# A gated linear attention: causal mask moved from TensorE to POOL, carry weights broadcast by DMA, bias halves in two PSUM banks, output gate rows loaded earlier

## The chip, the cores and the metric

The kernel runs on one core of one Trainium2 chip. The metric is the device time of one launch in microseconds (us). A core has the engines PE (TensorE, matrix products), ACT (ScalarE), DVE (VectorE) and POOL (GpSimd), the queue SP that issues most transfers, and 16 DMA engines. SBUF is its working memory with 128 partitions, PSUM holds the results of PE in eight banks.

## The reference, cut to what matters

Four batches times eight heads (32 heads in all), 768 steps, 40 columns a head. A recurrent attention with exponential gates is followed by a layer with eight experts (one per token) and a gated network. The change touches the first part alone:

```
for t in range(S):
    m_new  = maximum(f[:, :, t] + m, i[:, :, t])
    f_stab = exp(f[:, :, t] + m - m_new);  i_stab = exp(i[:, :, t] - m_new);  m = m_new
    C = f_stab * C + i_stab * outer(v[t], k[t])
    n = f_stab * n + i_stab * k[t]
    h = C @ q[t];  denom = maximum(abs(n @ q[t]), 1)
    y[t] = sigmoid(o_gate[t]) * h / denom
x = y as (3072 tokens, 320 columns)      # then experts, then the last network
```

## The kernel before

The 768 steps are cut into 6 groups of 128 (`NC`), and one chunk is one group of one batch: 24 chunks (`NT`), numbered n = 4 c + b. Inside a chunk the recurrence is written as attention: weights exp(bias) between keys and queries, times the products of q and k, times v; what came before the chunk enters through a state per head, faded by a carry weight.

**Rows.** DVE scans the gates of a group (`rows_scan`), ACT and DVE split them into high and low parts (`rows_high`, `rows_low`), SP stores them to DRAM (`rows_store`) and loads them back as operands: `bias_key` and `bias_carry` by group (`group_rows`), `bias_query` by chunk (`query_rows`). A bias product has 18 rows: the low and high key parts times ones, ones times the query parts. The rows that pick a head are a 0/1 pattern made by POOL in `bias_query[0]` and copied by ACT for the other three batches (L686).

**PE.** `front(n)`: the carry product (L1293, from the second group on) writes carry weights to the bank `CARRY`; then for each half of the heads a bias product (L1298) into the one bank `BIAS` and a product of the bf16 identity with a constant mask (L1299) that adds -1e30 where a key comes after the query; between the halves the scores (L1306). `increments(n)` (L1319) makes the new state, `head_columns(n)` (L1330) turns the outputs to tokens and makes the logits, `gate_turn(n)` (L1279) transposes the output gate rows into `BIAS`, `attend(n)` multiplies the state by qa (L1344) and v by the weights (L1353). The order by hand, turn i of the loop at L1387: front(i+1), increments(i), in one turn of four the ranks of a group, head_columns(i-1), gate_turn(i+2), attend(i). "Turn" below is this.

**ACT.** Turn i: `outputs(i-1)` copies the outputs (L679), `weights(i+1, h)` takes the exponentials of both halves (L660), `decayed` copies the last carry column (L666), `gates(i+2)` applies the gate (L672, L674).

**DVE.** Turn i: floor of the denominators of chunk i-2, `carry(i+1)` (qa = q times the carry weights in PSUM, L876), reciprocal, `scaled(i-2)` (L920, L922), `probs(i+1, 0)` (weights times scores, L883), `head_sum`, `update(i)` of the state (L896), `probs(i+1, 1)`. Every fourth turn it also scans rows, or chooses experts, or ranks.

**POOL.** Turn i: `gated_heads(i-1)` (zT, L605), `fade(i)` (L597), `weigh(i+1)` (L589), and from turn 8 on `scatter(i-8)`, which sends finished rows to DRAM in the order of the experts (L612).

**SP.** For each chunk `loads(n)` waits until chunk n-4 is done, then issues the gate rows `og_tok`, q and k, and k and v by tokens, and `query_rows(n)`; in one of four it stores and reloads the rows of a group.

The single bank `BIAS` is passed on: half 0, half 1, gate rows, each written only when ACT has read the one before (`weights_ready`, `tanh_ready`). Before the loop PE zeroes some banks, runs 14 products on constants so as to be busy (`keep_warm`), and runs front(0) and gate_turn(1).

```
def front(n):                                            # cut
    pe.wait_ge(tanh_ready, n + 1)
    for h in range(2):
        if h:
            pe.wait_ge(weights_ready, 2 * n + 1)
        mm(BIAS, bias_key, bias_query, stop=False)       # L1298
        mm(BIAS, ident16[:], maskT[:], start=False)      # L1299
        if h == 0:
            ...                                          # scores, L1306
```

## Time and profile before

| what | value |
|---|---|
| runs | 908.79, 911.25, 911.15 us; median 911.15 |
| the profiled execution | 914.29 us, its span 912.5 us, mean granted clock 0.964 |
| PE busy | 849.8 us (93%), 6301 products |
| DVE, ACT, POOL busy | 509.3, 394.0, 110.7 us |
| DMA | 109.37 MB, mean 120 GB/s |
| attention part | to about 190 us of the span |
| first bias product, last attend | 15.99 us, 184.16 us |

The span runs from the first to the last instruction of one profiled execution; 1.8 us of that execution lie around it. The executions that were only timed took up to 0.6% less. Busy times of several engines overlap. "Granted clock" is the share of 2.4 GHz that the chip let PE run at. In a timeline row the first number is the start, the second how long the instruction was busy, and brackets tell how long the engine stood idle before it and what released it.

### The profile page before, as it was taken

Reading aid. Unit: us, or ns where it says so; the run is one execution under the profiler, and the core shown is the slowest. Engines: PE = TensorE matmul, PEld = TensorE weight load, DVE = VectorE, ACT = ScalarE, POOL = GpSimd, SP = SyncE. Lnnn points to the kernel's source line nnn. Section 1 sums busy time; section 2 is a strip of 40 time slices with the busy share of each in tenths; the row PEclk is TensorE's granted clock in tenths of the full one; section 3 lists DMA queues with packets and bytes.
Section 4 is the critical chain, followed back from the end, with each engine's and each line's share of the span. In section 5 each row is a group of like instructions: output and inputs, shape, how many; then the busy total and the mean of one; then the engine's idle time right before and its main releaser. Section 6 shows DMA issues by size and latency. Waiting matters only on the chain.

```text
span 912.5 us, 18039 instructions
## 1 busy us (share of the span) xinstructions
PE 849.8 (93%) x6301; PEld 743.1 (81%) x6301; DVE 509.3 (56%) x1060; ACT 394.0 (43%) x714; POOL 110.7 (12%) x151
## 2 busy tenths in 40 slices
PE   5999999915999999999994999999999999999997
PEld 2777777615999999999993788888888888888886
DVE  4466566555788787878772344354354354453432
ACT  4444444404777767677761232232232233233122
POOL 4234454340000000000001100100100100100000
PEclk8899999966999999999997999999999999999999
DMA  6354445258889999999961100100100100100000
GB/s 166 89 146 129 147 140 165 72 200 279 251 266 262 266 269 279 264 253 291 296 203 37 30 1 1 58 1 1 58 0 0 58 0 0 58 0 2 28 1 29
DMA packets 76567, 109.37 MB, mean 120 GB/s; under 512 B 11380, under 2 KB 55284, under 8 KB 76516
## 3 DMA queue, kind: packets, MB, share of 16 engines
q1 hardware_dynamic: 72036, 98.20, 36.7%
q0 software_dynamic: 2304, 7.88, 2.6%
q10 hardware_dynamic: 2176, 2.62, 0.9%
q8 instruction: 30, 0.49, 0.2%
q14 instruction: 21, 0.17, 0.1%
HBM read 92.21 MB, written 16.47 MB: 119 GB/s over the span
## 4 chain that ended last, share of the span: by engine, by line
PE 85%; issue 5%; DMA 3%; ACT 2%; POOL 2%; DVE 1%; ACTq 1%; SPq 1%; POOLq 0%; DVEq 0%
PE psum L1419 42%; PE psum L1494 5%; PE psum L1495 5%; PE psum L1496 5%; PE psum L1443 4%; PE psum L1445 4%; PE psum L1444 4%; PE psum L1279 3%; PE psum L1330 2%; PE psum L1353 2%; PE psum L1306 2%; PE psum L1298 2%; PE psum L1299 1%; DMA w_raw<-w 1%; PE psum L1411 1%
## 5 line engine op out<-in xcount | busy, mean ns | idle before, releaser
L1242 DVE TENSOR_TENSOR gated_lo<-gated,gated_hi 128x512 fp32r<-128x512 f32 x72 | 49.9, 693 | 185.7 <-ACT gated_hi L807 185.7
L802 ACT ACTIVATE sigm_sb<-psum 128x512 f32<-128x512 f32 x72 | 43.0, 598 | 255.8 <-PE psum L1419 255.8
L1419 PE MATMUL psum<-nT_hi,w_gv_hi 128*128 128x512 f32 x432 | 125.1, 398 | 2.6 <-DVE nT_lo L1229 2.6
L1419 PE MATMUL psum<-nT_lo,w_gv_hi 128*128 128x512 f32 x432 | 124.5, 396 | 0.0
L1419 PEld LDWEIGHTS psum<-nT_lo,w_gv_hi 128*128 128x128 f32 x432 | 81.5, 189 | 19.9
L1419 PEld LDWEIGHTS psum<-nT_hi,w_gv_hi 128*128 128x128 f32 x432 | 79.0, 189 | 16.9 <-DVE nT_lo L1229 2.8
L1419 PE MATMUL psum<-nT_hi,w_gv_lo 128*128 128x512 f32 x288 | 90.6, 396 | 0.0
L635 POOL DMA_INDIRECT c_rows<-y_by_slot,slot_idx x24 | 22.8, 948 | 555.8 <-DMA y_by_slot<-y_tile 286.3
L1494 PE MATMUL psum<-w_out_hi,gated_hi 128*128 128x320 f32 x288 | 89.8, 312 | 0.0
L1495 PE MATMUL psum<-w_out_lo,gated_hi 128*128 128x320 f32 x288 | 89.1, 309 | 0.0
L1496 PE MATMUL psum<-w_out_hi,gated_lo 128*128 128x320 f32 x288 | 89.0, 309 | 0.0
L1419 PE MATMUL psum<-xT_hi,first_hi 128*128 128x256 f32 (+1 forms) x456 | 79.3, 283 | 2.0 <-DVE xT_lo L1095 2.0
L1443 PE MATMUL psum<-second_hi,hT_hi 128*128 128x320 f32 x248 | 78.4, 316 | 1.5 <-DVE hT_lo L1116 1.5
L1419 PE MATMUL psum<-xT_lo,first_hi 128*128 128x256 f32 (+1 forms) x456 | 79.1, 283 | 0.0
L1445 PE MATMUL psum<-second_hi,hT_lo 128*128 128x320 f32 x248 | 76.7, 309 | 0.0
L1444 PE MATMUL psum<-second_lo,hT_hi 128*128 128x320 f32 x248 | 76.7, 309 | 0.0
L723 ACT ACTIVATE second_hi<-w_raw 128x640 fp32r<-128x640 f32 x76 | 54.4, 737 | 36.8 <-PE psum L1445 33.6
L717 ACT ACTIVATE first_hi<-w_raw 128x1536 fp32r<-128x1536 f32 x38 | 56.6, 1490 | 29.4 <-DMA w_raw<-w 29.4
L1419 PEld LDWEIGHTS psum<-xT_hi,first_hi 128*128 128x128 f32 x456 | 66.5, 195 | 2.4 <-DVE xT_lo L1095 2.4
L1110 DVE TENSOR_TENSOR second_lo<-w_raw,second_hi 128x640 fp32r<-128x640 f32 x76 | 59.3, 822 | 11.8 <-ACT second_hi L723 11.2
L1419 PEld LDWEIGHTS psum<-xT_lo,first_hi 128*128 128x128 f32 x456 | 65.9, 195 | 0.0
L1419 PEld LDWEIGHTS psum<-nT_hi,w_gv_lo 128*128 128x128 f32 x288 | 54.2, 188 | 13.4
(222 smaller groups left out, 1571.5 us busy)
## 6 DMA issues: line engine op xcount, KB each, us to landing
w_raw<-w SPq DMA_DIRECT2D x38, 640.0 KB, 6.9
w_raw<-w SPq DMA_DIRECT2D x38, 512.0 KB, 4.5
w_raw<-w SPq DMA_DIRECT2D x76, 128.0 KB, 5.1
kv_tok<-tok SPq DMA_DIRECT2D x24, 324.0 KB, 4.4
qk_sb<-qk SPq DMA_DIRECT2D x48, 160.0 KB
y_by_slot<-y_tile SPq DMA_DIRECT2D x12, 321.0 KB, 7.3
og_tok<-o_tok SPq DMA_DIRECT2D x24, 160.0 KB, 2.2
x_tile<-x_by_expert SPq DMA_DIRECT2D x12, 320.0 KB, 2.9
```

The costliest lines, as they stand in the source:

```text
L717: nc.scalar.activation(first_hi[:, :, c], w1_raw[:, :, c], ACT.Copy).then_inc(w1_hi, 1)
L723: nc.scalar.activation(second_hi[:, 2 * r:2 * r + 2], w2_raw[:, 2 * r:2 * r + 2], ACT.Copy).then_inc(w2_hi, 1)
L802: nc.scalar.activation(sigm_sb[f % 2][:], bank[2 * (f % 2)][:], ACT.Sigmoid).then_inc(sig_ready, 1)
L1110: dve.tensor_tensor(second_lo[:, f], w2_raw[:, f], second_hi[:, f].bitcast(F32), ALU.subtract).then_inc(w2_lo, 1)
L1242: dve.tensor_tensor(gated_lo[f % 4][:], gated[f % 2][:], gated_hi[f % 4][:].bitcast(F32), ALU.subtract).then_inc(hv_lo, 1)
L1419: m = mm(dst, w, x, start=(n == 0), stop=(n == len(terms) - 1))
L1443: mm(o, hT_hi[:, r, c], second_hi[:, f], start=(f == 0), stop=False)
L1444: mm(o, hT_hi[:, r, c], second_lo[:, f], start=False, stop=False)
L1445: m = mm(o, hT_lo[:, r, c], second_hi[:, f], start=False, stop=(f == NF1 - 1))
L1494: mm(o, gated_hi[f % 4][:, c], w_out_hi[:, f], start=(f == 0), stop=False)
L1495: mm(o, gated_hi[f % 4][:, c], w_out_lo[:, f], start=False, stop=False)
L1496: m = mm(o, gated_lo[f % 4][:, c], w_out_hi[:, f], start=False, stop=(f == NF2 - 1))
```

## The change

Six edits that hang together:

1. The two mask products go, with `ident16`, `maskT` and `zero16`. A new POOL step `mask(n, h)` sets prob_T to zero where the key comes after the query, in place, after DVE has written it. Attend waits for `probs_masked`.
2. The carry product, the bank `CARRY`, `parity`, `bias_carry` and ACT's `decayed` go. The carry row is kept as one f32 row (`parts[:, 4]`), stored with the others, and for each chunk `carry_rows(n)` loads it with two broadcast DMAs (64 and 40 partitions, 4 rows of 512 bytes each) into `carry[b]`. DVE (`carried`) and POOL (`fade`) read it from SBUF.
3. The bias halves get a bank each. The gate rows share the second. The scores come after both bias products.
4. `gate_load(n)` takes the gate rows' load out of `loads`; it waits for the gate turn of chunk n-4 and is issued two chunks ahead. gate_turn and gates run three chunks ahead instead of two; there are four `gate` tiles.
5. The head pattern is a small tile (16x8) that ACT expands for each batch (`selected`); `group_rows(1)` comes before the router's weights.
6. Before the loop PE starts on a tile zeroed by DVE, runs 6 warm products, then three gate turns with 2 warm products behind each, then front(0).

```diff
                     sp.wait_ge(qk_cleared, n + 1)
                 else:
                     sp.wait_ge(chunk_done, n - B + 1)
-                sp.dma_start(og_tok[b][:, 0:DM], o_tok[i * P:(i + 1) * P, :]).then_inc(og_in[b], 16)
                 for r in range(2):
                     sp.dma_start(qk_sb[b][64 * r:64 * r + D].rearrange("p w a t -> p (w a t)"),
                                  qk[i * 2 * D + r * D:i * 2 * D + (r + 1) * D, :]).then_inc(qk_in[b], 16)
                 sp.dma_start(kv_tok[b][:], tok[i * P:(i + 1) * P, :]).then_inc(tok_in[b], 16)
+
+            def gate_load(n):
+                c, b = divmod(n, B)
+                i = b * NC + c
+                wait(sp, og_ready, n - B + 1)
+                sp.dma_start(og_tok[b][:, 0:DM], o_tok[i * P:(i + 1) * P, :]).then_inc(og_in[b], 16)
+
+            def carry_rows(n):
+                c, b = divmod(n, B)
+                wait(sp, qa_ready, n - 2 * B + 1)
+                wait(sp, state_faded, n - 2 * B + 1)
+                for r in range(2):
+                    w = 64 if r == 0 else D
+                    sp.dma_start(carry[b][64 * r:64 * r + w],
+                                 row_dram[c, 4, b * H:(b + 1) * H].rearrange("(a r) t -> r a t", r=2)[r].partition_broadcast(w)).then_inc(carry_in[b], 16)
...
             def rows_store(c):
-                k = 6 if c else 4
-                sp.wait_ge(rows_ready, 2 + 3 * c)
+                k = 5 if c else 4
+                sp.wait_ge(rows_ready, 2 * c + 2)
+                wait(sp, row_exp, c)
                 sp.dma_start(row_dram[c, 0:k].rearrange("n r t -> r n t"), parts[c % 2][:, 0:k].bitcast(F32)).then_inc(rows_out, 16)
...
-                if c:
-                    for r in range(2):
-                        sp.dma_start(bias_carry[c % 2][2 * r:2 * r + 2].bitcast(F32),
-                                     row_dram[c, 4:6].rearrange("n (k r) t -> r n k t", r=2)[r]).then_inc(carry_in[c % 2], 16)
...
             sp.wait_ge(pads_made, 1)
+            gate_load(0)
             loads(0)
+            gate_load(1)
+            gate_load(2)
             loads(1)
             rows_store(0)
             group_rows(0)
-            query_rows(0)
-            query_rows(1)
+            for n in range(B):
+                query_rows(n)
             loads(2)
             loads(3)
-            query_rows(2)
-            query_rows(3)
             rows_store(1)
+            for n in range(3, 6):
+                gate_load(n)
+            group_rows(1)
             sp.wait_ge(head_out_made, 1)
...
             sp.dma_start(rms_gain[:], rms_g.partition_broadcast(P)).then_inc(gain_in, 16)
-            group_rows(1)
             for n in range(B, NT):
+                carry_rows(n)
                 loads(n)
                 query_rows(n)
+                if n + 2 < NT:
+                    gate_load(n + 2)
                 if n % B == 2 and n // B + 1 < NC:
                     rows_store(n // B + 1)
                     group_rows(n // B + 1)
...
+            def mask(n, h):
+                pool.wait_ge(probs_ready, 2 * n + h + 1)
+                t = prob_T[n % 2][:, h]
+                pool.affine_select(out=t, in_=t, compare_op=ALU.is_ge, fill=0.0, base=0,
+                                   pattern=[[0, HH], [1, P]], channel_multiplier=-1).then_inc(probs_masked, 1)
...
             def fade(n):
                 c, b = divmod(n, B)
-                pool.wait_ge(decay_ready, n - B + 1)
...
                 pool.tensor_tensor(faded[n % 2][q], state[(c - 1) % 2][b][q],
-                                   decay[n % 2][q].unsqueeze(2).to_broadcast([64 + D, HP, D1]), ALU.mult).then_inc(state_faded, 1)
+                                   carry[b][q, :, P - 1:P].to_broadcast([64 + D, HP, D1]), ALU.mult).then_inc(state_faded, 1)
...
+            mask(0, 0)
             weigh(0)
+            mask(0, 1)
             constants()
             for i in range(NT + 1):
                 if i >= 1:
                     gated_heads(i - 1)
                 if B <= i < NT - B:
                     fade(i)
+                if i + 1 < NT:
+                    mask(i + 1, 0)
                 if i + 1 < NT - B:
                     weigh(i + 1)
+                if i + 1 < NT:
+                    mask(i + 1, 1)
                 if i >= 2 * B:
                     scatter(i - 2 * B)
...
                 if c:
-                    nc.scalar.activation(row_a[:], row_mu[:], ACT.Exp, bias=row_start[:, c:c + 1], scale=-1.0).then_inc(row_exp, 1)
-                    act.wait_ge(row_exp, c)
-                    nc.scalar.activation(a_hi, row_a[:], ACT.Copy).then_inc(row_high, 1)
+                    nc.scalar.activation(parts[c % 2][:, 4].bitcast(F32), row_mu[:], ACT.Exp, bias=row_start[:, c:c + 1], scale=-1.0).then_inc(row_exp, 1)
+
+            def selected(b):
+                nc.scalar.activation(bias_query[b][0:2 * H], select[:].unsqueeze(2).to_broadcast([2 * H, H, P]), ACT.Copy).then_inc(select_copied, 1)
...
-                nc.scalar.activation(exp_weight[n % 2][:, h].rearrange("p a t -> p (a t)"), BIAS, ACT.Exp).then_inc(weights_ready, 1)
-
-            def decayed(n):
-                act.wait_ge(qa_ready, n - B + 1)
-                wait(act, state_faded, n - B - 1)
-                q = slice(0, 64 + D)
-                nc.scalar.activation(decay[n % 2][q], CARRY.rearrange("p (a t) -> p a t", a=HP)[q, :, P - 1], ACT.Copy).then_inc(decay_ready, 1)
+                nc.scalar.activation(exp_weight[n % 2][:, h].rearrange("p a t -> p (a t)"), BIAS[h], ACT.Exp).then_inc(weights_ready, 1)
...
                 act.wait_ge(og_ready, n + 1)
-                wait(act, z_ready, n - 2)
-                t = gate[n % 3][0:M2]
-                nc.scalar.activation(t, BIAS[0:M2], ACT.Tanh, scale=gate_rows[0:M2, 0:1]).then_inc(tanh_ready, 1)
+                wait(act, z_ready, n - 3)
+                t = gate[n % 4][0:M2]
+                nc.scalar.activation(t, BIAS[1][0:M2], ACT.Tanh, scale=gate_rows[0:M2, 0:1]).then_inc(tanh_ready, 1)
...
+            act.wait_ge(select_made, 1)
+            selected(0)
             rows_high(0)
             act.wait_ge(gate_rows_made, 1)
             gates(0)
-            act.wait_ge(select_made, 1)
-            for b in range(1, B):
-                nc.scalar.activation(bias_query[b][0:2 * H], bias_query[0][0:2 * H].bitcast(F32), ACT.Copy).then_inc(select_copied, 1)
+            selected(1)
+            gates(1)
+            selected(2)
+            gates(2)
             rows_high(1)
             for h in range(2):
                 weights(0, h)
-            gates(1)
+            selected(3)
...
                     weights(i + 1, 1)
-                if i + 2 < NT:
-                    gates(i + 2)
+                if i + 3 < NT:
+                    gates(i + 3)
...
-            def carry(n):
-                b = n % B
-                dve.wait_ge(qk_in[b], 32 * (n // B) + 32)
-                dve.wait_ge(carry_ready, n - B + 1)
+
+            def carried(n):
+                c, b = divmod(n, B)
+                dve.wait_ge(qk_in[b], 32 * c + 32)
+                dve.wait_ge(carry_in[b], 32 * c)
                 wait(dve, chunk_done, n - 1)
                 q = slice(0, 64 + D)
                 dve.tensor_tensor(qa[n % 2][q].rearrange("p a t -> p (a t)"), qk_sb[b][q, 0].rearrange("p a t -> p (a t)"),
-                                  CARRY[q], ALU.mult).then_inc(qa_ready, 1)
+                                  carry[b][q].rearrange("p a t -> p (a t)"), ALU.mult).then_inc(qa_ready, 1)
...
+            dve.memset(warm16[:], 0.0).then_inc(dve_made, 1)
+            dve.memset(ones16[:], 1.0).then_inc(dve_made, 1)
...
             def gate_turn(n):
                 b = n % B
                 pe.wait_ge(og_in[b], 16 * (n // B) + 16)
-                wait(pe, weights_ready, 2 * n)
+                wait(pe, weights_ready, 2 * n - 2 if n >= 3 else 0)
+                wait(pe, tanh_ready, n)
...
+                            m = mm(BIAS[1][64 * o:64 * o + 64, s * P:(s + 1) * P], og_tok[b][:, h * D:h * D + 64], ident[:], start=True, stop=True)
...
+                if c == 0:
+                    pe.wait_ge(select_copied, b + 1)
                 pe.wait_ge(query_in[b], 16 * c + 16)
-                if c:
-                    wait(pe, qa_ready, n - B)
-                    wait(pe, decay_ready, min(n - B, NT - 2 * B))
-                    mm(CARRY, parity[:], bias_carry[p][:, b * HP:(b + 1) * HP].rearrange("r a t -> r (a t)"), start=True, stop=True).then_inc(carry_ready, 1)
-                pe.wait_ge(tanh_ready, n + 1)
                 for h in range(2):
+                    wait(pe, weights_ready, 2 * n - 1 + h)
                     if h:
-                        pe.wait_ge(weights_ready, 2 * n + 1)
-                    mm(BIAS, bias_key[p][:, b], bias_query[b][:].rearrange("r (a q) t -> r q a t", q=2)[:, h], start=True, stop=False)
-                    mm(BIAS, ident16[:], maskT[:].rearrange("p a t -> p (a t)"), start=False, stop=True).then_inc(bias_ready, 1)
-                    if h == 0:
-                        pe.wait_ge(qk_in[b], 32 * c + 32)
-                        wait(pe, probs_ready, 2 * n)
-                        for a in range(HH):
-                            for g in range(2):
-                                r = slice(64 * g, 64 * g + D)
-                                m = mm(SCORES[g][:, a * P:(a + 1) * P], qk_sb[b][r, 1, a], qk_sb[b][r, 0, a], start=True, stop=True)
-                                if a == HH - 1:
-                                    m.then_inc(scores_ready, 1)
+                        pe.wait_ge(tanh_ready, min(max(n + 2, 3), NT))
+                    mm(BIAS[h], bias_key[p][:, b], bias_query[b][:].rearrange("r (a q) t -> r q a t", q=2)[:, h], start=True, stop=True).then_inc(bias_ready, 1)
+                pe.wait_ge(qk_in[b], 32 * c + 32)
+                wait(pe, probs_ready, 2 * n)
+                for a in range(HH):
+                    for g in range(2):
+                        r = slice(64 * g, 64 * g + D)
+                        m = mm(SCORES[g][:, a * P:(a + 1) * P], qk_sb[b][r, 1, a], qk_sb[b][r, 0, a], start=True, stop=True)
+                        if a == HH - 1:
+                            m.then_inc(scores_ready, 1)
 
...
-                pe.wait_ge(probs_ready, 2 * n + 2)
+                pe.wait_ge(probs_masked, 2 * n + 2)
...
             pe.wait_ge(dve_made, 2)
-            pe.wait_ge(mask_made, 2)
             for r in range(2):
-                mm(OUT_T[:, r], zero16[:], maskT[:].rearrange("p a t -> p (a t)"), start=True, stop=True)
-            mm(STATE, zero16[:], maskT[:].rearrange("p a t -> p (a t)"), start=True, stop=True)
+                mm(OUT_T[:, r], ones16[:], warm16[:], start=True, stop=True)
+            mm(STATE, ones16[:], warm16[:], start=True, stop=True)
+            keep_warm(6)
             pe.wait_ge(ident_made, 1)
-            gate_turn(0)
-            keep_warm(14)
-            pe.wait_ge(mask_made, 3)
-            pe.wait_ge(select_copied, B - 1)
+            for n in range(3):
+                gate_turn(n)
+                keep_warm(2)
             front(0)
-            gate_turn(1)
...
-                if i + 2 < NT:
-                    gate_turn(i + 2)
+                if i + 3 < NT:
+                    gate_turn(i + 3)
```

## Rows read from the trace of the kernel before

**Rows 1.** Busy time by stretch; columns: engines' busy us (instructions), PEclk, DMA share, GB/s

```profile
31.46:50.15 18.69, 18.47 (x232) 13.97 (x230) 9.10 (x26) 9.33 (x20) 6.06 (x6) 0.99 0.50 141
50.15:162.27 112.12, 111.76 (x1511) 81.19 (x1509) 70.34 (x225) 53.72 (x108) 50.76 (x59) 1.00 0.48 143
106.31:113.25 6.94, 6.94 (x95) 5.05 (x93) 4.92 (x14) 3.17 (x6) 3.44 (x4) 1.00 0.52 154
113.25:120.39 7.14, 7.02 (x96) 5.05 (x94) 4.82 (x17) 4.03 (x10) 3.44 (x4) 1.00 0.47 142
```

**Rows 2.** Timeline of one turn, PE; columns: start us, busy us, instruction

```profile
155.33 0.49 PE L1293 MATMUL psum<-bias_carry,parity 4*128 4x512 f32 x1
...
155.66 0.40 PE L1298 MATMUL psum<-bias_query,bias_key 18*128 18x512 f32 x1
...
156.31 1.16 PE L1306 MATMUL psum<-qk_sb 40*128 40x128 f32 x16
...
157.40 0.50 PE L1298 MATMUL psum<-bias_query,bias_key 18*128 18x512 f32 x1
...
158.15 0.51 PE L1319 MATMUL psum<-v_weighted,kv_tok 128*40 128x41 f32 x16
...
159.66 1.09 PE L1279 MATMUL psum<-ident,og_tok 128*64 128x128 f32 x16
```

**Rows 3.** Timeline of the same turn, ACT, POOL and DVE

```profile
155.44 0.60 ACT L679 ACTIVATE oT<-psum 105x512 f32<-105x512 f32 x1 [0.23 <-PE psum L1353]
...
155.91 0.69 DVE L876 TENSOR_TENSOR qa<-qk_sb,psum 104x512 f32<-104x512 f32 x1 [2.92 <-PE psum L1293]
...
156.13 1.26 POOL L605 TENSOR_TENSOR zT<-oT,gate 105x512 f32<-105x512 f32 x1 [2.30 <-ACT oT L679]
...
157.36 0.28 DVE L922 TENSOR_TENSOR logit_parts<-psum,inv_denom 128x128 f32<-128x128 f32 x1
...
158.94 0.68 DVE L883 TENSOR_TENSOR prob_T<-exp_weight,psum 128x512 f32<-128x512 f32 x1
```

**Rows 4.** Timeline of a late turn without bias products, PE

```profile
179.40 1.08 PE L1353 MATMUL psum<-prob_T,kv_tok 128*41 128x128 f32 x16
...
182.51 1.15 PE L1330 MATMUL psum<-head_out,zT 105*128 105x114 f32 x8 [2.04 <-POOL zT L605]
```

**Rows 5.** The line of the old constant mask: duration ns min/median/max

```profile
L546 POOL TENSOR_SCALAR_AFFINE_SELECT maskT<-maskT x1: 642/642/642, 7.6 to 7.6; 128x512 bf16<-128x512 bf16 x1
```

**Rows 6.** One DVE line (ns min/median/max), and the timeline at its longest

```profile
L865 DVE SCALAR_TENSOR_TENSOR parts<-row_mu,parts x6: 271/272/1162, 6.2 to 125.1; 32x128 fp32r<-32x128 f32 x6
...
4.85 2.36 POOL L540 TENSOR_SCALAR_AFFINE_SELECT bias_query<-bias_query 16x1024 fp32r<-16x1024 f32 x2
...
6.19 1.16 DVE L865 SCALAR_TENSOR_TENSOR parts<-row_mu,parts 32x128 fp32r<-32x128 f32 x1
```

**Rows 7.** Queue 1 from 10.2 to 12.8, then 80 to 160 us: packets, MB, share

```profile
q1 hardware_dynamic: 88, 0.05, 6.5%
...
q1 hardware_dynamic: 5411, 10.25, 44.4%
```

**Rows 8.** Timeline of the start

```profile
11.42 0.55 SPq L365 DMA_DIRECT2D bias_query<-gate_rows  x2
...
12.96 2.93 ACT L686 ACTIVATE bias_query<-bias_query 16x1024 fp32r<-16x1024 f32 x3
...
22.51 0.76 PE L1298 MATMUL psum<-bias_query,bias_key 18*128 18x512 f32 x1 [0.87 <-ACT gate L672]
...
31.46 0.63 PE L1298 MATMUL psum<-bias_query,bias_key 18*128 18x512 f32 x1
```

**Rows 9.** Busy time and granted clock in two stretches of 1 us, columns as in rows 1

```profile
18.00:19.00 1.00, 0.88 (x2) 0.10 (x1) 0.69 (x2) 0.08 (x1) 0.00 (x0) 0.56 1.02 298
31.00:32.00 1.00, 1.00 (x7) 0.37 (x3) 0.00 (x0) 0.64 (x2) 0.00 (x0) 0.61 0.00 0
```

**Rows 10.** DMA issues on the page: KB each, us to landing

```profile
og_tok<-o_tok SPq DMA_DIRECT2D x24, 160.0 KB, 2.2
```

75 lines of the change are left out of this document (23 added, 52 removed).

## The prediction

> **What bounds the kernel now.** I read the busy time by stretch first, because the change touches only the recurrent attention part, which runs up to about 190 us of the 912.5 us span. In the 16 full loop turns between 50.15 and 162.27 us PE is busy 111.76 of 112.12 us, at full clock; in one turn of 6.94 us PE has 6.94, DVE 4.92, ACT 3.17 and POOL 3.44 us, and the DMA engines are busy for 0.52 of it [rows 1]. So a turn lasts as long as PE's list of work, and the other engines have room. Then I read one turn of PE in order of time, by starts, since a start-to-start distance is what an instruction really costs: carry product to first bias 0.33, first bias with its mask to the scores 0.65, second bias with its mask to the state increments 0.75 [rows 2]. Next the chain beside PE: the ACT copy of the outputs starts 0.11 after the turn starts (I count from the carry product at 155.33), the POOL product zT 0.80 after it and lasts 1.26, DVE's qa runs at 0.58, its last reading of the head columns starts 2.03 after, its second prob_T starts 3.61 after [rows 3]. Where PE has nothing to put in between, the head columns start 3.11 after the last products of a chunk start; these take 1.00 by starts, so the floor is about 2.1 us from a turn's start to its head columns [rows 4].
>
> **The steady turns.** The change takes three matmuls out of a turn: the carry product and the two mask products. A product of this size takes 0.33 by starts, as the carry product shows. So 0.33 goes with it, 0.65 - 0.33 = 0.32 with the first mask and 0.75 - 0.34 = 0.41 with the second, 1.06 in all; I use 1.05 [rows 2]. A turn becomes 6.94 - 1.05 = 5.89. The head columns come after two bias products, the scores (1.09) and the increments (row of 0.51, some 0.43 by starts): 0.34 + 0.34 + 1.09 + 0.43 = 2.20 from the turn's start, against the floor of 2.1. That fits by 0.1 us, so PE still sets the turn, but any delay of zT now lands on it. Over turns 4 to 19 the sum is 16 x 1.05 = 16.8. In three of these turns ACT's row work held up the second bias, because both halves share a bank: the turn at 113.25 lasts 7.14 with PE busy 7.02 [rows 1]. With two banks this goes: 3 x 0.2 = 0.6.
>
> **POOL** gets two masks a turn. The nearest row is the old constant mask, the same select over 128x512 elements: 0.64 [rows 5]. It is bf16 there and f32 now, so the upper bound is POOL's two-input 512-element product, 1.26 [rows 3]; I take 0.65, since the operation is the same. POOL's list is then 3.44 + 1.30 = 4.74 of 5.89. In order: zT 0.80 to 2.06, fade to 2.5, first mask from about 2.65 (after prob_T) to 3.3, weigh to 4.05, second mask to 4.7, scatter to about 5.85; the next zT is due at 6.69. Covered, with 0.8 us to spare. Attend of a chunk needs masks made in the turn before, so their latency is hidden.
>
> **DVE** multiplies qa from a carry tile in SBUF instead of PSUM; I leave the price at 0.69, and it may start at 0.12 rather than 0.58 as no product precedes it. Its list of 4.92 fits in 5.89. But one row speaks against this. DVE's 271 ns instruction on parts took 1162 ns once: exactly while POOL's 16x1024 select ran, and it ended with it [rows 6]. Both its inputs lie in SBUF. So a DVE operation with two SBUF inputs waits for POOL, and qa becomes one. At 0.12 to 0.81 it ends just as zT starts (0.80), which costs nothing. In turns with a row scan or an expert choice the first two-input step also meets a mask, so DVE ends some 0.65 later and qa may push zT by 0.1 to 0.2: 8 turns x 0.15 = 1.2 us lost. The Trainium skill, page SBUF — State Buffer, section Who interferes with whom, says that a DVE instruction with two SBUF inputs and a GpSimd instruction that reads SBUF block each other for the whole instruction; the trace agrees (1162 against 271 ns), and without such a rule the sum would be 1.2 us better.
>
> **DMA.** Two small carry loads per group go; each chunk from the fifth on gets two broadcast loads, 416 rows of 512 bytes. Two bounds for a packet: 6.5% x 16 x 2.6 us / 88 = 31 ns in a stretch of small ones, and 44.4% x 16 x 80 us / 5411 = 105 ns in the loop's average, where rows are bigger [rows 7]. So 26 packets per engine add 0.8 to 2.7 us to 0.52 x 6.94 = 3.6 us: 4.4 to 6.3 of a 5.89 us turn. I take the low end (nearest in size), no stall, and keep 0.7 us for the unevenness. SP issues about three more DMAs of 0.3 to 0.7 us in a turn; it waits for PE most of the time, and the loads are still issued two turns ahead. The gate rows' loads leave the wait on chunk_done for one on an older gate turn; their matrix turn keeps its place in PE's list, one chunk earlier.
>
> Steady turns: 16.8 + 0.6 - 1.2 = 16.2 us.
>
> **Turns 1 to 3** last 18.69 us [rows 1]. They lose two masks each (0.72) and the last one the carry product, 2.5, with the bank wait 2.8. **The last turns** (20 to 22) lose 1.05 each, but with no increments the head columns would come at 1.77, so the floor of 2.1 takes back 0.34: 2.1. One gate turn (row of 1.09, 1.0 by starts) leaves for the prologue. DVE's choice at turn 21 now ends after PE wants qa; I charge 1.3. Net 1.8.
>
> **Prologue.** Now: the bias rows are issued at 11.42, but the first bias also waits for three ACT copies that end at 15.89; the next chunk's bias starts at 22.51 after the gate tanh, the one after at 31.46 [rows 8]. The granted clock falls from 1.00 to 0.56 at 18 to 19 us, and is back only in 31 to 32 us [rows 9], so all of turn 0 runs at 1.2 of 2.4 GHz. After: ACT's copies (2.93 for three) and the gates of three chunks, estimated at 4 us from about 4.5 on, are done by about 12, so the first bias waits for the rows only. One more og load (160 KB, 0.6 us at the 298 GB/s of [rows 9]) is ahead of them: issued at 12.0, landed 2.2 later as an og load does [rows 10], first bias at 14.2. PE has idled about 3 us by then, so I assume the low clock again, at which a bias takes 0.76 [rows 8] and the rest double. front(0) is 1.5 + 2.2 = 3.7, two biases of chunk 1 end at 19.4, scores 2.2 (21.6), increments 0.9, gate turn 2.0, attend 2.0 less what the returning clock gives: about 26.1, against 31.46, a gain of 5.4. The masks and weigh of chunk 0 (some 2 us after its scores) lie under it.
>
> **Sum:** 5.4 + 2.8 + 16.2 + 1.8 - 0.7 (DMA) = 25.5 us. Routing tables, experts and the last network start earlier by this and do not change. The profiled run took 914.29 us, the median of the runs is 911.15, 0.34% less. 914.29 - 25.5 = 888.8 on the profiled execution, 911.15 - 25.5 = 885.7 on the median; I say 885.7.
>
> **Rivals.**
> (1) The f32 mask costs 1.26. POOL: zT at 0.80, masks and weigh to 5.9, scatter to 7.1, so a turn of 6.3 in the 12 with a scatter: 12 x 0.4 = 5, time 890. For it: f32 operands; against: the same select at 0.64. Chance 0.10.
> (2) The DMA engines bound at 6.3 a turn: 20 x 0.4 = 8, time 893. For it: 105 ns is the loop's own average; against: 31 ns for small ones. Chance 0.13. Ending on the other side: from 94 ns a packet on (26 x 94 ns = 2.4 us) the turn is no shorter than 6.0, and at 105 + 90 ns, if 64 readings of the same row cost as much again, it is 8.7, and 20 turns x 1.8 = 36 us lost against some 9 won outside these turns: 938, slower. It decides from about 150 ns a packet on (26 x 150 ns = 3.9, turn 7.5), where twenty turns lose those 9 us. Against it: 31 ns. Chance 0.04.
> (3) qa and zT collide: in nine turns with scan or choice DVE comes after 0.80, zT goes first, qa ends at 2.75, the head columns slip from 2.2 to 3.85: 9 x 1.65 = 15, time 900. For it: [rows 6] and the 0.7 us of slack; against: DVE's list of 4.92. Chance 0.09.
> (4) The clock does not fall: turn 0 ends some 4 us earlier still, 882. Chance 0.08.
> (5) The removed matmuls were hidden and nothing moves: PE busy all the turn speaks against it. Chance 0.02.
> My forecast has 0.54. The range reaches over rivals 1, 2's first case and 4, and takes in most of 3.
>
> **Numbers.** Range 877 to 899. About 0.3% is what a measurement can tell from no change. Faster 0.93 (all but rival 5 and the slow end of 2), same 0.02, slower 0.05 (that end, and 0.01 for what I have not seen).
>
> **What would show it.** Right: turns of 5.9 us at clock 1.00, PE busy over 0.97, select rows near 0.65, head columns 2.2 after a turn's start, first bias near 14, turn 1 starting near 26. Wrong: PE idle before head columns with zT as releaser (POOL or the port), before biases or scores with a DMA as releaser, qa or zT rows stretched beyond 0.69 and 1.26, a DMA share above 0.9.

## The result and the profile after

The changed kernel takes 884.93 us (median of 4 runs, 883.98 to 888.20), beside 911.20 us for the kernel before on the same chip: ratio 0.9706, 95% interval 0.968 to 0.9733 (the quotient of the two medians is 0.9711). The profiled execution took 885.66 us (span 883.9 us, mean granted clock 0.962) against 914.29 us, 28.6 us less. Below are the stretches that answer to [rows 1]: turns 1 to 3, turns 4 to 19, turns 20 to 22, then one turn alone; columns as there.

```profile
25.56:41.66 16.10, 15.62 (x224) 12.98 (x222) 9.19 (x25) 8.51 (x18) 9.72 (x12) 1.00 0.80 200
41.66:136.47 94.81, 94.51 (x1462) 75.26 (x1460) 75.03 (x222) 48.70 (x90) 70.20 (x91) 1.00 0.75 204
136.47:152.22 15.75, 14.69 (x197) 11.34 (x195) 12.53 (x39) 6.04 (x11) 10.38 (x12) 1.00 0.25 78
95.03:100.90 5.87, 5.87 (x92) 4.67 (x90) 5.16 (x17) 3.55 (x8) 4.69 (x7) 1.00 0.95 278
```

Sixteen turns now take 94.81 us where they took 112.12, and PE is still busy all but 0.30 us of it. POOL went from 3.2 to 4.4 us a turn on average (in a single turn with a scatter from 3.44 to 4.69, forecast 4.74), and the DMA engines from 0.48 to 0.75 of the time, in single turns 0.95. One turn in order of time, PE first (a turn with the rank products, 5.99 us), then ACT, DVE and POOL; it answers to [rows 2, 3]:

```profile
100.90 0.73 PE L1296 MATMUL psum<-bias_query,bias_key 18*128 18x512 f32 x2
101.56 1.16 PE L1302 MATMUL psum<-qk_sb 40*128 40x128 f32 x16
...
103.23 1.13 PE L1326 MATMUL psum<-head_out,zT 105*128 105x114 f32 x8
104.29 1.09 PE L1281 MATMUL psum<-ident,og_tok 128*64 128x128 f32 x16
...
105.89 1.07 PE L1349 MATMUL psum<-prob_T,kv_tok 128*41 128x128 f32 x16
101.02 0.60 ACT L680 ACTIVATE oT<-psum 105x512 f32<-105x512 f32 x1 [0.23 <-PE psum L1349]
101.12 0.69 DVE L877 TENSOR_TENSOR qa<-qk_sb,carry 104x512 f32<-104x512 f32 x1 [0.43 <-PE psum L1349]
101.71 1.27 POOL L605 TENSOR_TENSOR zT<-oT,gate 105x512 f32<-105x512 f32 x1 [0.90 <-ACT oT L680]
...
103.57 0.64 POOL L579 TENSOR_SCALAR_AFFINE_SELECT prob_T<-prob_T 128x512 f32<-128x512 f32 x1 [0.17 <-DVE prob_T L884]
...
104.88 0.69 POOL L579 TENSOR_SCALAR_AFFINE_SELECT prob_T<-prob_T 128x512 f32<-128x512 f32 x1
105.73 1.01 POOL L612 DMA_INDIRECT x_by_expert<-y_tok,x_row  x1 [0.16 <-issue]
```

The two bias products stand back to back and no mask follows. The selects lie where the working put them, and POOL stands still for no more than 0.17 us at a time except for the 0.90 us before zT. The start, on PE, and the two stretches that show the clock fall and return, answer to [rows 8, 9]:

```profile
13.85 0.69 PE L1296 MATMUL psum<-bias_query,bias_key 18*128 18x512 f32 x2 [2.24 <-DMA bias_query<-gate_rows]
...
22.12 1.98 PE L1281 MATMUL psum<-ident,og_tok 128*64 128x128 f32 x16 [1.76 <-DMA og_tok<-o_tok]
23.89 1.75 PE L1349 MATMUL psum<-prob_T,kv_tok 128*41 128x128 f32 x16
25.56 0.73 PE L1296 MATMUL psum<-bias_query,bias_key 18*128 18x512 f32 x2
```

```profile
15.00:16.00 1.00, 1.00 (x13) 0.78 (x9) 0.00 (x0) 1.00 (x2) 0.00 (x0) 0.54 0.85 276
25.00:26.00 1.00, 1.00 (x10) 0.65 (x6) 0.00 (x0) 0.81 (x2) 0.05 (x1) 0.84 0.14 8
```

PE still stands still for 2.24 us, then the lower level (1.2 of 2.4 GHz) holds through chunk 0, as before, but turn 1 begins at 25.56 instead of 31.46 us.

### The profile page after: what moved, and what is told of

Its sections match the earlier page's. It is cut to its first block, busy times and chain, and to the rows that moved or that the text cites. A ratio compares the mean times of both kernels' runs of the same rounds, so it can differ in the third digit from the quotient of the medians.

```text
span 883.9 us, 17960 instructions
## 1 busy us (share of the span) xinstructions
PE 825.1 (93%) x6231; PEld 733.6 (83%) x6231; DVE 512.2 (58%) x1055; ACT 388.0 (44%) x694; POOL 135.2 (15%) x190
## 4 chain that ended last, share of the span: by engine, by line
PE 86%; DMA 4%; issue 3%; DVE 2%; POOL 2%; ACT 2%; SPq 1%; ACTq 1%; DVEq 0%; POOLq 0%
PE psum L1413 45%; PE psum L1488 5%; PE psum L1489 5%; PE psum L1490 5%; PE psum L1437 4%; PE psum L1439 4%; PE psum L1438 4%; PE psum L1281 2%; PE psum L1326 2%; PE psum L1349 2%; PE psum L1302 2%; PE psum L1296 1%; PE psum L1340 1%; PE psum L1405 1%; PE psum L1469 1%
```

## The experiments

"The changed kernel" is taken as 0.9706 of the kernel before, which was timed again beside the runs of each experiment: some 885 to 887 us. Its turns are those of the profile above.

**Each mask made twice** (the changed kernel):

```diff
-                                   pattern=[[0, HH], [1, P]], channel_multiplier=-1).then_inc(probs_masked, 1)
+                                   pattern=[[0, HH], [1, P]], channel_multiplier=-1).then_inc(masked_once, 1)
+                pool.wait_ge(masked_once, 2 * n + h + 1)
+                pool.affine_select(out=t, in_=t, compare_op=ALU.is_ge, fill=0.0, base=0,
+                                   pattern=[[0, HH], [1, P]], channel_multiplier=-1).then_inc(probs_masked, 1)
```

> The changed kernel with each POOL select run twice (the second changes nothing). Theory A, POOL's masks lie beside PE's work with 0.8 us to spare in a turn of 5.87: two more selects of 0.64 make POOL's list about 6.3 us in the 12 turns with a scatter, so those turns take 6.3 and the kernel 5 us more, about 890; turns without a scatter stay at 5.87. Theory B, attend waits for the masks or DVE is held up by them every turn: 1.3 us more in all 23 turns, 30 us, about 915. Theory C, POOL has far more room: no change, 885.

Measured: 899.69 us, ratio 0.9861 (0.9828 to 0.9894), about 15 us over the changed kernel: between the two theories. Plain turns without a scatter kept 5.87 us. Of the twelve turns with one, the last eight took 6.19 to 6.34, which is 2.4 us in all, A's step but less of it. By the profile the last head columns start 14.8 us later than in the changed kernel; 1.0 more comes from turn 11 (6.83 us, a wait of 0.90), and some 12 from turn 1 (9.15 us for 5.17), turn 9 (10.33) and the last two turns (3.5 together), all at the lower level; 0.5 was won before turn 1. Turn 1 ran at the lower level in kernels with an untouched start too (last section), so its 4 us can't be put down to the masks. Turn 9 on PE, then the stretch of 1 us behind its wait:

```profile
78.44 2.05 PE L1330 MATMUL psum<-head_out,zT 105*128 105x114 f32 x8 [1.34 <-POOL zT L609]
80.42 1.97 PE L1285 MATMUL psum<-ident,og_tok 128*64 128x128 f32 x16
```

```profile
79.00:80.00 1.00, 1.00 (x6) 1.00 (x6) 0.97 (x4) 0.00 (x0) 0.93 (x2) 0.50 0.69 253
```

Products of 1.15 and 1.09 us take 2.05 and 1.97 here. POOL's slack is real: a scatter turn has 1.3 us more of POOL's work and takes 0.3 more, so about 1.0 us was free, where 0.8 was forecast. But a wait is not priced by its own length.

**The carry broadcasts twice** (the changed kernel):

```diff
+        carry_more = [sb(f"carry_more{b}", [P, HP, P], F32, ga) for b in range(B)]
...
+                    sp.dma_start(carry_more[b][64 * r:64 * r + w],
+                                 row_dram[c, 4, b * H:(b + 1) * H].rearrange("(a r) t -> r a t", r=2)[r].partition_broadcast(w)).then_inc(more_in[b], 16)
```

> The changed kernel with the two carry broadcasts of each chunk from the fifth on issued a second time, into tiles that nobody reads. The changed kernel's DMA share from 60 to 136 us is about 0.75 and each pair of broadcasts added some 1.1 us of engine time to a turn. Theory A, transfers are issued two turns ahead and the queue has room: share about 0.9, time within 2 us of 885. Theory B, the DMA engines are at their limit: a turn becomes 6.3 or more, PE waits for q and k or for the gate rows, 8 us or more slower, 893 and up.

Measured: 908.96 us, ratio 0.998 (0.9955 to 1.0005): 24 us more, as B has it; nearly the whole gain of the change is gone. The DMA share from 60 to 65 us is 1.04, and PE's longest waits in the loop (2.57, 1.82 and 1.42 us) are for rows that come late; another, 1.54 us, is for DVE's logit_parts. Behind the wait of 1.82 us (PE's timeline, then the stretch behind it) the clock was 0.50 and the turn took 8.98 us:

```profile
83.44 0.73 PE L1303 MATMUL psum<-bias_query,bias_key 18*128 18x512 f32 x2 [1.82 <-DMA bias_query<-gate_rows]
```

```profile
85.00:90.00 5.00, 5.00 (x51) 4.41 (x49) 2.97 (x8) 0.06 (x1) 3.00 (x4) 0.50 0.98 228
```

The run doubles the loads and SP's issues of them together, and the trace shows both behind this wait. SP may issue the query rows of this turn only after the stored rows of the next group have landed: it waited 7.4 us for those, in the changed kernel 5.1. Then it took 4.8 us for the issues of a chunk instead of 3.2, and the query rows went out 3.8 us before the turn wants them, in the changed kernel 7.0. How the 24 us divide between the two stays open. The run does say that the change left little room on that path.

**The masks alone moved** (the kernel before, with the selects on POOL and no mask product; carry product, shared bank and start as they were; the new POOL step is that of the change):

```diff
...
-                    mm(BIAS, bias_key[p][:, b], bias_query[b][:].rearrange("r (a q) t -> r q a t", q=2)[:, h], start=True, stop=False)
-                    mm(BIAS, ident16[:], maskT[:].rearrange("p a t -> p (a t)"), start=False, stop=True).then_inc(bias_ready, 1)
+                    mm(BIAS, bias_key[p][:, b], bias_query[b][:].rearrange("r (a q) t -> r q a t", q=2)[:, h], start=True, stop=True).then_inc(bias_ready, 1)
...
-                pe.wait_ge(probs_ready, 2 * n + 2)
+                pe.wait_ge(probs_masked, 2 * n + 2)
```

> The kernel before with one part of the change: the two mask products go and POOL's select takes their place; carry product, single bank and start stay. Theory A, PE's list sets the turn: 0.73 us less in 23 turns, 16 to 17 us, about 894.5, turns of 6.2. Theory B, the single bank's chain (bias, exponential, bias, gate rows) or the chain to zT takes over once PE is shorter: a gain below 8 us, above 903, PE idle before its second bias or before the head columns.

Measured: 906.10 us, ratio 0.9921 (0.9893 to 0.995): 6 us gained, not 16. The plain turn did nearly what A says, 6.30 us for 6.94 (A has 6.2). But with the mask product gone, PE reaches the second bias before ACT has emptied the bank: in the four turns in which ACT makes the row parts (1, 5, 9 and 13) it waits 0.67, 0.45, 0.74 and 0.73 us. Behind the first and the last of these the lower level follows, with turns of 8.71, 8.94 and 8.71 us; behind the wait of 0.74 us it does not. Turn 13, its stretch, and then the same of turn 9:

```profile
111.08 0.50 PE L1311 MATMUL psum<-bias_query,bias_key 18*128 18x512 f32 x1 [0.73 <-ACT exp_weight L673]
...
111.94 2.00 PE L1342 MATMUL psum<-head_out,zT 105*128 105x114 f32 x8
```

```profile
113.00:115.00 2.00, 2.00 (x17) 1.80 (x18) 1.64 (x8) 0.00 (x0) 1.82 (x3) 0.50 0.19 62
```

```profile
84.96 0.50 PE L1311 MATMUL psum<-bias_query,bias_key 18*128 18x512 f32 x1 [0.74 <-ACT exp_weight L673]
```

```profile
85.00:87.00 2.00, 2.00 (x27) 1.60 (x29) 1.97 (x7) 0.60 (x1) 1.42 (x3) 1.00 0.86 229
```

**The masks back on PE** (the changed kernel with the mask product behind each bias and no select on POOL, else as it is):

```diff
...
+                    mm(BIAS[h], ident16[:], maskT[:].rearrange("p a t -> p (a t)"), start=False, stop=True).then_inc(bias_ready, 1)
...
-                pe.wait_ge(probs_masked, 2 * n + 2)
+                pe.wait_ge(probs_ready, 2 * n + 2)
```

> The changed kernel with the mask part undone: mask products back on PE in both banks, no select on POOL. Theory A: turns of 6.6 us, 15 to 17 us slower than the changed kernel, about 900; it keeps 10 to 12 us against the kernel before, from the carry product (20 x 0.33) and the start (5.9). Theory B, the masks on POOL cost time that the trace hides: less than 10 us slower, below 895.

Measured: 901.94 us, ratio 0.9898 (0.9843 to 0.9952): 17 us over the changed kernel, turns of 6.70 us (6.83 with ranks), A's answer. That is 0.83 us a turn, 0.25 of it time in which PE stands idle before its second bias. What is left of the gain, 9 to 10 us, is what the carry product, the second bank and the start bring together; no run undoes the carry product or the new start by itself. So the same edit is worth 17 us with the rest of the change and 6 us without it.

**qa behind zT** (the changed kernel; DVE waits for ACT's copy and clears a small tile first, so that zT always starts before qa):

```diff
-                wait(dve, chunk_done, n - 1)
+                wait(dve, oT_copied, n - 1)
+                dve.memset(late[:], 0.0)
```

> The changed kernel with qa's start moved behind zT's: DVE waits for the copy of the outputs instead of the end of attend, and clears a small tile first, so qa comes about 0.95 us after a turn's start and zT 0.80. Theory A, a DVE operation with two SBUF inputs is shut out while POOL reads SBUF: qa ends at about 2.8 instead of 1.65, the head columns start at about 3.85 instead of 2.2, turns of about 7.5, 20 x 1.65 = 33 us slower, near 918. Theory B, they run side by side: qa ends at 1.65, its last reading of the head columns at 2.7, turns of 6.4, about 10 us slower, near 895. The qa rows tell it too: 0.69 or stretched to 1.8.

Measured: 955.24 us, ratio 1.0448 (1.0421 to 1.0475): 70 us over the changed kernel, twice what A has. The collision itself is as A prices it. Duration of qa in ns (min/median/max) here, then in the changed kernel, then one turn and one stretch here:

```profile
L879 DVE TENSOR_TENSOR qa<-qk_sb,carry x20: 1627/1634/1644, 41.0 to 218.0; 104x512 f32<-104x512 f32 x20
```

```profile
L877 DVE TENSOR_TENSOR qa<-qk_sb,carry x19: 691/692/693, 41.9 to 147.7; 104x512 f32<-104x512 f32 x19
```

```profile
79.14 1.27 POOL L606 TENSOR_TENSOR zT<-oT,gate 105x512 f32<-105x512 f32 x1 [4.76 <-ACT oT L681]
79.33 1.63 DVE L879 TENSOR_TENSOR qa<-qk_sb,carry 104x512 f32<-104x512 f32 x1
82.14 2.02 PE L1328 MATMUL psum<-head_out,zT 105*128 105x114 f32 x8 [1.54 <-DVE logit_parts L925]
```

```profile
80.00:85.00 5.00, 3.46 (x36) 3.08 (x34) 4.55 (x13) 0.04 (x1) 3.23 (x5) 0.64 0.58 173
```

qa, 0.69 us by itself, ends 0.55 us after zT's end; POOL's fade behind it is stretched in turn, from 0.46 to 0.91. The Trainium skill, page SBUF — State Buffer, section Who interferes with whom, has DVE's second port shared with GpSimd as an exclusive lock, and this pair of rows agrees. PE waits for logit_parts 20 times, 30.6 us together, the longest 2.2. At full clock a turn takes 7.45 us, as A has it; the other half of the 70 us is the clock, with turns of 10.2 to 10.3 us where the lower level follows the wait. It does not always follow:

```profile
161.32 1.12 PE L1328 MATMUL psum<-head_out,zT 105*128 105x114 f32 x8 [1.54 <-DVE logit_parts L925]
```

```profile
162.00:164.00 2.00, 2.00 (x38) 1.53 (x37) 1.81 (x7) 0.49 (x1) 1.84 (x4) 1.00 0.11 35
```

**The gate rows of turn 3 loaded sooner**, and, by itself, **12 zero products in place of 2 after the third gate turn** (the changed kernel both times):

```diff
             loads(2)
+            gate_load(3)
             loads(3)
```

```diff
                 gate_turn(n)
-                keep_warm(2)
+                keep_warm(2 if n < 2 else 12)
```

> The changed kernel with the gate rows of chunk 3 loaded before q, k and v of chunk 3 instead of after the stored rows; PE stood idle 1.76 us for them at 22.12. Theory A: they land some 3 us earlier, PE saves up to 1.7 us, about 883.3. Theory B, the masks of chunk 0 or the returning clock come next: below 0.5 us.

> The changed kernel with 12 warm products instead of 2 behind the third gate turn, so PE is busy from 11.0 to about 13.6 where it now idles 2.24 us. Theory A, the idle time before the first bias lets the clock fall at 15 us: it stays at 2.4 GHz, turn 0 ends some 4 us earlier, about 881. Theory B, the clock falls for the sparse work since the start or regardless: it falls near 15 us as well, no change beyond 0.5 us.

Measured: 886.01 us, ratio 0.9698 (0.9677 to 0.9719), and 886.19 us, ratio 0.9703 (0.9674 to 0.9732): neither can be told from the changed kernel, B's answer both times. In the first, attend of chunk 0 comes at 21.23 instead of 23.89 us, but PE then waits 1.03 us for head_out, the clock falls again, and turn 2 starts at 30.95 for 30.73. In the second the clock holds to 17 us instead of 15 and the turns stand 1 us earlier, 24.56 for 25.56.

**One bank for both bias halves** (the changed kernel, scores between the halves again):

```diff
...
-                    wait(pe, weights_ready, 2 * n - 1 + h)
+                    wait(pe, weights_ready, 2 * n + h)
...
-                    mm(BIAS[h], bias_key[p][:, b], bias_query[b][:].rearrange("r (a q) t -> r q a t", q=2)[:, h], start=True, stop=True).then_inc(bias_ready, 1)
+                    mm(BIAS[1], bias_key[p][:, b], bias_query[b][:].rearrange("r (a q) t -> r q a t", q=2)[:, h], start=True, stop=True).then_inc(bias_ready, 1)
```

> The changed kernel with both bias halves in one bank again: the second product waits for ScalarE's exponential of the first half, with the scores between them as before the change; the carry broadcasts, the masks on Pool and the early gate rows stay. Theory A (the second bank is what lets the rest of the change stand, because in the turns in which ScalarE makes the row parts first the second bias product waits 0.7 us and the granted clock then falls): 12 us or more over the changed kernel, about 897, with a TensorE wait on exp_weight near 0.7 us in four turns and turns of 7 to 10 us behind them. Theory B (the forecast's own term of 0.6 us): at most 3 us over it, about 888, and every turn under 6.3 us.

Measured: 890.47 us, ratio 0.9762 (0.9728 to 0.9795): 5 us over the changed kernel, nearer to B. Plain turns take 6.07 us, 0.20 more, and not because of ACT: the exponential of the first half ends at 61.47, before PE wants the bank. By starts the two products apart take 0.42 and 0.43 us, back to back they took 0.66:

```profile
60.27 0.49 PE L1296 MATMUL psum<-bias_query,bias_key 18*128 18x512 f32 x1
60.69 1.16 PE L1304 MATMUL psum<-qk_sb 40*128 40x128 f32 x16
...
61.78 0.50 PE L1296 MATMUL psum<-bias_query,bias_key 18*128 18x512 f32 x1
...
62.21 0.51 PE L1317 MATMUL psum<-v_weighted,kv_tok 128*40 128x41 f32 x16
```

Four turns also wait 0.31 to 0.46 us for ACT before the second bias (three of them take 6.46 to 6.60 us, the first 5.84), and none was followed by a lower clock. So the second bank is worth 5 us, and it does not by itself explain the 11 us between the two mask runs; I had expected it to.

**Three short waits put into PE** and **three longer ones** (the changed kernel; ACT makes a copy of k x 128 elements in turns 8, 12 and 16, and PE waits for it ahead of the gate turn; the longer ones have 27, 32 and 39 for 15, 19 and 24):

```diff
+        LATE = {8: 15, 12: 19, 16: 24}
...
+                if i in LATE:
+                    k = LATE[i]
+                    act.wait_ge(weights_ready, 2 * i + 4)
+                    wait(act, slow_made, list(LATE).index(i))
+                    nc.scalar.activation(slow[:, 0:k], ident[:].unsqueeze(1).to_broadcast([P, k, P]), ACT.Copy).then_inc(slow_made, 1)
...
+                if i in LATE:
+                    pe.wait_ge(slow_made, list(LATE).index(i) + 1)
```

> The changed kernel with one extra ScalarE copy in three turns (8, 12 and 16), which TensorE waits for ahead of the gate product; the copies are of 15, 19 and 24 x 128 elements, so that by ScalarE's rows the waits come out near 0.3, 0.8 and 1.3 us. Nothing else changes. Theory A (a wait of this size costs more than itself, because the granted clock falls behind it): the two longer ones make their turns or the next one 3 us longer each, the short one costs only its length; the kernel loses 6 to 8 us, about 892. Theory B (a wait costs its own length): 2.4 us in all, about 887.5, every turn under 7.3 us and the clock at 1.00 from 27 to 150 us.

> As the run with three short waits, with longer copies: 27, 32 and 39 x 128 elements in turns 8, 12 and 16, so that TensorE waits about 1.6, 2.1 and 2.9 us there (1.26 us were measured for 24 x 128, and 107 ns for each 128 more). The three short waits cost their own length and the granted clock stayed at 1.00; in the run with each mask twice a wait of 1.34 us was followed by 0.50. Theory A (a longer wait is followed by the lower clock level): the clock falls to 0.50 behind at least two of the three, each adds about 3.1 us to its wait (turn of 10.33 us in place of 5.87 with a wait of 1.34 there), and the kernel loses 13 to 16 us over the changed one, about 900. Theory B (a wait that stands alone costs its own length): 6.6 us, about 892, and the clock at 1.00 from 27 to 150 us.

Measured: 887.92 us, ratio 0.9724 (0.9696 to 0.9752), 2.2 us over the changed kernel, B's answer; and 901.63 us, ratio 0.9891 (0.9859 to 0.9923), 16.6 us over it, A's. The three waits of the short run on PE and the clock behind two of them, then the same of the long run:

```profile
69.56 1.09 PE L1290 MATMUL psum<-ident,og_tok 128*64 128x128 f32 x16 [0.24 <-ACT slow L712]
94.56 1.09 PE L1290 MATMUL psum<-ident,og_tok 128*64 128x128 f32 x16 [0.73 <-ACT slow L712]
120.17 1.09 PE L1290 MATMUL psum<-ident,og_tok 128*64 128x128 f32 x16 [1.26 <-ACT slow L712]
```

```profile
96.00:98.00 2.00, 2.00 (x31) 1.28 (x22) 0.84 (x4) 1.73 (x5) 0.43 (x2) 1.00 0.79 207
122.00:124.00 2.00, 2.00 (x28) 1.44 (x26) 0.97 (x3) 1.97 (x5) 0.38 (x1) 1.00 0.79 185
```

```profile
74.03 1.48 PE L1290 MATMUL psum<-ident,og_tok 128*64 128x128 f32 x16 [1.52 <-ACT slow L712]
101.94 1.98 PE L1290 MATMUL psum<-ident,og_tok 128*64 128x128 f32 x16 [2.12 <-ACT slow L712]
130.75 1.97 PE L1290 MATMUL psum<-ident,og_tok 128*64 128x128 f32 x16 [2.87 <-ACT slow L712]
```

```profile
74.00:76.00 2.00, 1.97 (x28) 1.62 (x32) 0.83 (x4) 0.44 (x1) 1.21 (x1) 0.65 0.92 254
132.00:134.00 2.00, 2.00 (x28) 1.28 (x26) 0.00 (x0) 1.20 (x2) 0.00 (x0) 0.50 0.07 22
```

Waits of 0.24, 0.73 and 1.26 us cost 2.2 us together, which is their sum (the interval of the run is 2.6 us to either side, so the exact match is luck; by the profile the three turns took 2.9 us more). Waits of 1.52, 2.12 and 2.87 us, 6.5 together, cost 16.6: each was followed by the lower level, and turns of 9.02, 9.78, 11.25 and, behind the last, 9.15 us make 15.7 of it. Such stretches also hold most of what the runs with doubled masks and with qa behind zT lost beyond the first step.

**The last products first** (the changed kernel; attend of the last chunk ahead of the head columns of the one before), and **that together with a mended start** (both edits of the start, the head weights' loads ahead of `loads(3)`, and 6 more zero products inside the second front):

```diff
+                if i == NT - 1:
+                    attend(i)
                 if i >= 1:
                     head_columns(i - 1)
...
-                if i < NT:
+                if i < NT - 1:
                     attend(i)
```

> The changed kernel, in which the products of the last turn (attend of 23) go ahead of the head columns of 22, which wait 2.0 us for zT. Theory A (the last products need only the masked probabilities and the copied OUT_T, both there 1 us before TensorE gets to them, and the end of the mixing part follows from them): they start near 153.1 us in place of 155.7, at full clock; the last head columns start near 157 in place of 160.7, and the kernel gains 3 to 4 us, about 881. Theory B (the expert part starts when its weights and rows have landed, whatever the mixing part does): within 0.5 us of the changed kernel, the first x transpose at 185.7 us as now.

> The last products first (as in the run before this one), and the start mended: the gate rows of turn 3 and the head weights are loaded behind the first two chunks of rows, 12 zero products stand behind the third gate turn and 6 more inside the second front. Theory A (the clock stays at 1.00 through the start, since TensorE no longer stands still there for 2.2 and 1.8 us, and the turns behind move up with it): turn 1 starts 2 us or more sooner than 25.6 us and the kernel gains 5 to 6 us over the changed one, about 879.5. Theory B (the start is bound by the first chunk's chain through VectorE and Pool, as the two earlier edits of the start showed): turn 2 starts where it does now, and the gain is that of the last products alone, about 881.

Measured: 886.68 us, ratio 0.9724 (0.9683 to 0.9766), and 884.47 us, ratio 0.97 (0.9674 to 0.9726): neither is told from 0.9706. Yet each edit does its part in its own place. PE in the second run, at the start and at the end:

```profile
21.52 0.73 PE L1297 MATMUL psum<-bias_query,bias_key 18*128 18x512 f32 x2
...
24.67 0.51 PE L1319 MATMUL psum<-v_weighted,kv_tok 128*40 128x41 f32 x16 [1.33 <-POOL v_weighted L590]
...
26.59 1.18 PE L1330 MATMUL psum<-head_out,zT 105*128 105x114 f32 x8 [1.41 <-POOL zT L606]
...
31.15 0.73 PE L1297 MATMUL psum<-bias_query,bias_key 18*128 18x512 f32 x2
...
149.30 0.73 PE L1297 MATMUL psum<-bias_query,bias_key 18*128 18x512 f32 x2
...
184.41 1.51 PE L1411 MATMUL psum<-ident,x_tile 128*128 128x128 f32 x6 [20.05 <-DMA x_tile<-x_by_expert]
```

The clock held through chunk 0, and turn 1 began at 21.52 us, 4 us sooner. Then PE stood still for POOL twice within 4 us: POOL makes its constant tables from 19.0 to 23.2 us, ahead of the masks of chunk 1; the clock fell (0.50 at 28 to 30 us), and turn 2 began at 31.15 where the changed kernel has 30.73. All 4 us were given back: the start is bound by POOL as well. At the end 35.1 us lie between the last front and the first x transpose, where the changed kernel has 185.66 - 147.07 = 38.6: 3.5 us won (the first of the two runs has 37.3; four runs with an untouched end, those with the edited start, one bank and short waits, have 39.1 to 40.9). The turns in between lost 1.8 of it, as told in the last section.

## Why the prediction was right

It said 885.7 us, and 884.93 were measured; on the profiled execution it said 888.8, and 885.66 were measured, a gain of 28.6 us for a forecast of 25.5. Step by step:

- **Steady turns**: forecast 5.89 us, measured 5.87; for sixteen of them 16.2 us of gain, measured 112.12 - 94.81 = 17.3. Taking PE's list by starts was right to 0.02 us a turn. The 1.2 us that I charged for collisions at the port did not come in these turns: all 19 recorded rows of qa took 691 to 693 ns. DVE's short operations on two SBUF inputs do stretch beside the selects (one of 191 ns takes 548), but nothing waits for them there. The split of the 1.05 us was less exact than its sum: the two masks, put at 0.73, are worth 0.64 a turn by themselves, the second bank, for which I had only ACT's wait, is worth 0.20, and that leaves 0.23 for the carry product, put at 0.33.
- **POOL**: select forecast at 0.65, measured 0.636 in f32 (median of 48, the longest 0.758). The first rival falls, and the doubled masks bear out the 0.8 us of slack: it was about 1.0.
- **Head columns**: forecast 2.2 us after a turn's start, measured 2.19. The margin of 0.1 us held in all plain turns, and was missed in turns 2, 3 and 4: there ACT's gate ends late, the copy of the outputs starts 0.50 after the turn's start instead of 0.12, and PE waits 0.23 to 0.24. Turns 1 to 3 so gained 2.6 in place of 2.8.
- **Turns 20 to 22**: 18.13 - 15.75 = 2.4 us, forecast 1.8; the terms without the charge for DVE's choice add up to 3.1, so of the 1.3 charged about half came. In turn 22 it came much as forecast: DVE's choice ends late, qa starts at 147.69, 0.6 after the turn, and zT, which starts beside it at 147.88, takes 1.64 us for 1.27.
- **Start**: first bias forecast at 14.2, measured 13.85; turn 1 forecast at 26.1, measured 25.56; gain 5.9 for 5.4. The clock fell as assumed, after 2.24 us without work for PE where I had said 3. Part of this gain is luck: the clock came back just as turn 1 began, while in three of five profiles with the same start it stayed low through turn 1 (last section). Not foreseen was the wait of 1.76 us for the gate rows of turn 3; loading them sooner gained nothing, so it had cover.
- **DMA**: this step came out near its low end, and its margin was the one I judged worst. The loop's share is 0.75; that is 4.4 us of a turn, the figure forecast, but by two misses that cancel: I started from the 3.6 us of one turn where the loop's mean was 3.4, and took 31 ns for a packet, where 0.75 x 5.93 - 0.48 x 7.0 = 1.1 us for 26 packets per engine is 42 ns each. The 0.7 us kept for unevenness did not come: no wait of PE for a DMA stands in turns 1 to 22. With the broadcasts doubled the gain is gone. I gave the second rival 0.13 + 0.04, and that run shows how near it was.
- **The end**: forecast unchanged. The clock fell earlier there, behind PE's wait of 2.04 us for zT in turn 23, and attend of the last chunk took 1.89 us for 1.08: 1.6 us lost.
- **Rival 3** happened once, in turn 22, in small; forced, it costs 3.5 us a turn, not 1.65: the term had the stretch right and left out the clock. **Rival 4** was made to happen by the last kernel: turn 0 did end 4 us earlier, and the 4 us were gone by turn 2.

The gains by the profile up to the last attend are 5.9 + 2.6 + 17.3 + 2.4 - 1.6 = 26.6 us of the 28.6; the remaining 2.0 lie behind, where I had forecast nothing: 1.2 before the first x transpose (26.2 us after the last head columns before, 25.0 now) and 0.8 in the experts. Against the forecast that makes +0.5 at the start, -0.2 in turns 1 to 3, +1.1, +0.6, +0.7 (DMA), -1.6 at the end and +2.0 behind, +3.1 in all. The mechanism was right for the reasons given. That the median was met to 0.8 us is closer than the working, and in part luck: the medians differ by 26.3 us where the profiled executions differ by 28.6, and the four runs of the changed kernel lie up to 4 us apart.

What was not priced is how the parts hang together. Each part was costed as if the others held: alone, the masks gain 6 us and not 16, because PE then waits for ACT in four turns and the lower level follows two of these waits; without them the rest gains 9 to 10. The sum is right for the whole only, since it leaves PE no wait above 0.5 us in turns 1 to 22.

## What to carry to other kernels

Where one engine is busy all the time, a turn can be priced closely (here to 0.02 us) by the distances between starts on it, and what a change is worth is right only if no new wait appears on that engine: cost each wait not by its length alone but with the stretch at the lower clock that can follow (here 1.6 to 5.8 us). Test the headroom by doubling the added work on each engine and queue: here POOL had it and the loads had not, which the time alone did not tell. An early start of one turn is worth nothing while the engine beside it is still behind: the same 4 us were won and given back.

## What was unexpected of the hardware

- **The clock behind a wait.** One wait of 1.26 us left the granted clock at 1.00, one of 1.52 was followed by 0.50, and in this kernel that costs 1.6 to 5.8 us besides the wait (turns of 9.02, 9.78 and 11.25 us for 5.87, the last with a next one of 9.15). Length alone does not settle it, in either direction: in the run with the masks alone a wait of 0.73 us was followed by 0.50 and one of 0.74 us, at the same place four turns sooner, by 1.00; in the run with qa behind zT a wait of 1.54 us was followed by 1.00. What else decides was not settled.
- **When the clock comes back.** Five profiles have the same start: the changed kernel and the runs with qa late, short waits, long waits and the last products first. In all the clock is low through chunk 0. In the changed kernel it is back at 26 us, and turn 2 begins at 30.73; with short waits at 31.17; in the other three it is low through turn 1, which takes 8.7 to 8.8 us, and turn 2 begins at 33.48 to 34.46. The stretch with the last products first:

```profile
26.00:28.00 2.00, 2.00 (x19) 1.78 (x20) 0.00 (x0) 1.13 (x3) 0.84 (x1) 0.50 0.38 125
```

So one profile of the start tells it only to some 3 us; why the clock comes back earlier in two of the five is open.
- **The same turn at two lengths.** In the changed kernel's profile the copy of the outputs starts 1.12 us after the last products begin, in every turn from 5 on to 19. In the last two kernels, whose loop is the same, it starts there at first, and from about 75 us on, in turns 9 to 19, mostly 1.3 to 1.6 us after; the runs with short and long waits, with the doubled broadcasts and with the masks alone have it in the same turns, the kernel before and the runs with doubled masks, masks on PE, and the two edits of the start do not. zT comes later by as much, PE waits for it, and turns take 6.03 to 6.28 us where they took 5.87 to 5.99. Over turns 2 to 21 that was 118.15 us against 116.34. PE's own records are alike in both, and what releases ACT later is open. With the start it may account for part of the spread of the runs (880.87 to 892.42 us for one kernel), which hides gains of 2 us; only one execution of each kernel was profiled, so that is not shown.
- **Small broadcast packets are cheap.** 42 ns for 512 bytes is between the 31 and 105 ns of [rows 7]; a share of 0.95 over a turn (95.03 to 100.90 us) was seen with PE busy for all of it.
